# First tile of the first MLP by plain products over 384 tokens at once, and a new order of the filling steps

## What is computed

```python
def _attn_ref(q, k, v, tau):
    qn = q / (np.linalg.norm(q, axis=1, keepdims=True) + 1e-06)
    kn = k / (np.linalg.norm(k, axis=1, keepdims=True) + 1e-06)
    s = kn.transpose(0, 2, 1) @ qn / tau            # 256 x 256
    a = np.exp(s - s.max(-1, keepdims=True))
    a /= a.sum(-1, keepdims=True) + 1e-09
    return v @ a

x = _attn_ref(q, k, v, tau).reshape(6016, 256)
h = x @ moe_w_in                                    # 256 -> 2048
x = (h * np.cos(h)) @ moe_w_out                     # 2048 -> 256
h = x @ moe2_w_in
y = (h * (1.0 / (1.0 + np.exp(-h)))) @ moe2_w_out
```

## Time and profile before

| | |
|---|---|
| median of 3 executions | 1026.3 us (1025.75 to 1026.33) |
| the profiled execution | 1024.68 us |
| its span in the profile | 1022.9 us |
| PE busy, 8718 matmuls | 1017.5 us, 99% |
| DVE busy | 945.7 us, 92% |
| ACT busy | 801.4 us, 78% |
| POOL busy | 1.5 us |

### The profile page before, as it was taken

How to read it: one execution, slowest core, us unless ns; L and a number is a source line. 1 busy time by engine, 2 the same in 40 slices (tenths; PEclk the granted TensorE clock), 3 DMA queues, 4 the chain that set the end, 5 groups by cost and what they waited for, 6 DMA issues and landing times.

```text
span 1022.9 us, 21208 instructions
## 1 busy us (share of the span) xinstructions
PE 1017.5 (99%) x8718; PEld 1006.9 (98%) x8718; DVE 945.7 (92%) x1062; ACT 801.4 (78%) x873; POOL 1.5 (0%) x14
## 2 busy tenths in 40 slices
PE   9999999999999999999999999999999999999998
PEld 9969999999999999999999999999999999999998
DVE  7999899999999999998988689999999999999987
ACT  7778778788788787787777677877877877878785
POOL 0000000000000000000000000000000000000000
PEclk9999999999999999999999999999999999999999
DMA  8830011230331312304145401101101101101000
GB/s 274 289 121 22 2 57 38 98 135 21 114 115 41 114 52 85 135 22 165 37 165 237 169 18 37 31 12 42 40 5 43 41 2 42 42 1 42 22 22 21
DMA packets 18701, 76.03 MB, mean 74 GB/s; under 512 B 1840, under 2 KB 6448, under 8 KB 16560
## 3 DMA queue, kind: packets, MB, share of 16 engines
q1 hardware_dynamic: 18608, 74.72, 21.2%
HBM read 47.71 MB, written 27.00 MB: 73 GB/s over the span
## 4 chain that ended last, share of the span: by engine, by line
PE 92%; ACT 0%; issue 0%; DVE 0%; ACTq 0%
PE banks L1442 31%; PE banks L1446 31%; PE banks L1445 31%; PE banks L1499 0%; ACT g_hi L571 0%; ACT s_part L524 0%; DVE xo L1161 0%; ACTq L570 0%; ACT banks L516 0%; ACTq L523 0%
## 5 line engine op out<-in xcount | busy, mean ns | idle before, releaser
L1445 PE MATMUL banks<-g_lo,w1out 128*128 128x256 f32 (+1 forms) x768 | 212.5, 277 | 0.0
L1442 PE MATMUL banks<-g_hi,w1out 128*128 128x256 f32 (+1 forms) x768 | 212.4, 277 | 0.0
L1446 PE MATMUL banks<-g_hi,w1out 128*128 128x256 f32 (+1 forms) x768 | 212.3, 276 | 0.0
L1442 PE MATMUL banks<-xf_hi,h1w 128*128 128x256 f32 (+1 forms) x672 | 187.6, 279 | 1.1 <-ACT banks L516 0.6
L1446 PE MATMUL banks<-xf_hi,h1w 128*128 128x256 f32 (+1 forms) x672 | 185.9, 277 | 0.0
L1445 PE MATMUL banks<-xf_lo,h1w 128*128 128x256 f32 (+1 forms) x672 | 185.9, 277 | 0.0
L1445 PE MATMUL banks<-xf_lo,h2w 128*128 128x256 f32 (+1 forms) x672 | 185.9, 277 | 0.0
L1442 PE MATMUL banks<-xf_hi,h2w 128*128 128x256 f32 (+1 forms) x672 | 185.8, 277 | 0.0
L1446 PE MATMUL banks<-xf_hi,h2w 128*128 128x256 f32 (+1 forms) x672 | 185.8, 276 | 0.0
L1445 PE MATMUL banks<-g_lo,o2w 128*128 128x256 f32 (+1 forms) x670 | 185.2, 276 | 0.0
L1446 PE MATMUL banks<-g_hi,o2w 128*128 128x256 f32 (+1 forms) x670 | 185.2, 276 | 0.0
(11 more groups left out here) (149 smaller groups left out, 2305.9 us busy)
## 6 DMA issues: line engine op xcount, KB each, us to landing
w_scr<-w_split SPq DMA_DIRECT2D x8, 1792.0 KB, 7.5
qk_raw<-qk SPq DMA_DIRECT2D x23, 512.0 KB, 4.4
h2w<-w_scr SPq DMA_DIRECT2D x4, 1792.0 KB, 8.0
o2w<-w_scr SPq DMA_DIRECT2D x4, 1792.0 KB, 8.0
form<-v_tiles SPq DMA_DIRECT2D x11, 512.0 KB, 3.6
x_scr<-xo SPq DMA_DIRECT2D x11, 512.0 KB, 2.6
form<-x_scr SPq DMA_DIRECT2D x11, 512.0 KB, 4.2
y_tiles<-xo SPq DMA_DIRECT2D x10, 512.0 KB, 5.1
```

Of the source, the lines that this page charges most:

```text
L1442: nc.tensor.matmul(out, w_hi, m_hi, start=start, stop=False, skip_group_check=True)
L1445: nc.tensor.matmul(out, w_hi, m_lo, start=False, stop=False, skip_group_check=True)
L1446: return nc.tensor.matmul(out, w_lo, m_hi, start=False, stop=stop, skip_group_check=True)
```

## The change

**First tile on PE.** Steps 0 to 3 no longer use the scheme. A unit u (`first_hidden`) is one group e of one step: u = 2q + e. It computes the plain product over both blocks of channels (k) for all 384 tokens: each matmul takes both halves, as two runs of 192 columns, and its result has the same two runs in one bank. A unit is 2 (groups of 128 features) x 2 (k) x 3 passes = 12 matmuls and fills two banks, 2(u mod 3) and the next. It waits until the unit three before has been gated (`unit_gated`), or, for u < 3, until the fold has left the banks. `first_output` has four groups a step of 6 matmuls, also over 384 columns, in place of eight groups over 192. Units 6 and 7 end with one extra matmul of 128 columns into the part of a bank that the first tile leaves unwritten.

**First tile on ACT and DVE.** Each unit has turns, phase, sine and gate of its own over 768 elements, all against PSUM: `first_turns`, `first_phase`, `first_sine`, `first_gate`. s1, s2, s3, c22 and c12 do not exist in steps 0 to 3. `hi_of_g` and `lo_of_g` are as before. The form of the first tile has no sums: four blocks of it are split instead of seven.

**Weights.** Slot 0 of the weights is now needed in two parts too: a new tensor `w11`. ACT moves each half of a fold whole to `wr[f]` (`move_fold`), then takes high parts from there (`hi_11`, `hi_three`); DVE makes `lo_11`, `lo_three` and the four sums, all from SBUF. The sums of fold f, with `hi_sums` and `lo_sums`, are first read in tile 1, steps 4 to 7.

**The rest.** `wr0` and `wr1` move in SBUF, `FOLD_BANKS`, `X_BANKS` and `OUT_AT` get other bank numbers, semaphores that count steps of the scheme start at step 4, and SP's first `load_raw` waits for the first tile's outputs and splits too. The hand-written lists of the filling are new on all three engines. From step 8 on the order is as before.

The core of the diff (`...` marks what is left out):

```diff
-        X_BANKS = (5, 6, 7)
+        X_BANKS = (6, 7, 5)
...
+        def unit_banks(u):
+            return banks[:, 2 * (u % 3):2 * (u % 3) + 2, :, 0:N[0]]
...
-        FOLD_BANKS = [(0, 1), (2, 3), (6, 7), (5, 7)]
+        FOLD_BANKS = [(0, 1), (2, 3), (4, 5), (6, 7)]
...
+                        for m in range(PIECES):
+                            sp.wait_ge(w_lo_ready[m], 1)
+                        sp.wait_ge(out_done[0], STEPS)
+                        sp.wait_ge(out_done[1], STEPS)
+                        sp.wait_ge(w11_ready, STEPS)
+                        sp.wait_ge(wu_three_ready, STEPS)
                         sp.wait_ge(h1w_sums_ready[3], 1)
...
+                def move_fold(f, k):
+                    act.wait_ge(fold_ready[k], f + 1)
                     act.wait_ge(row_scale_ready, 1)
+                    nc.scalar.activation(fold_slots(wr[f], 2 * k, 2 * k + 2), bank(FOLD_BANKS[f][k]), ACT.Copy,
+                                         scale=row_scale[:, k:k + 1]).then_inc(fold_moved[k], 1)
...
+                def first_turns(u):
+                    act.wait_ge(unit_done, u + 1)
+                    if u >= 4:
+                        act.wait_ge(g_lo_ready, u // 2 - 1)
+                    nc.scalar.activation(work_int[:, unit_slots(u), :, 0:N[0]], unit_banks(u), ACT.Identity,
+                                         bias=0.25).then_inc(unit_turns, 1)
...
+                def lo_three(f):
+                    dve.wait_ge(wu_three_hi, f + 1)
+                    nc.vector.tensor_tensor(h1w[f][:, 1, 0:3, :, :], wr[f][:, 1:4, :, :], h1w[f][:, 0, 0:3, :, :],
+                                            ALU.subtract).then_inc(wu_three_ready, 1)
...
-                    if f == 3 and k == 1:
-                        pe.wait_ge(wu_slot7, 3)
-                        pe.wait_ge(h1w_raw_ready[2], 2)
...
+                def first_hidden(u):
+                    q, e = divmod(u, 2)
+                    pe.wait_ge(xf_ready, 1)
+                    if e == 0:
+                        pe.wait_ge(w11_ready, q + 1)
+                    pe.wait_ge(wu_three_ready, q + 1)
+                    if u < 3:
+                        pe.wait_ge(fold_moved[0], u + 1)
+                        pe.wait_ge(fold_moved[1], u + 1)
+                    else:
+                        pe.wait_ge(unit_gated, u - 2)
+                    for j in range(2):
+                        for k in range(KC):
+                            w_hi, w_lo = (h1w[q][:, part, 2 * k + e - 1, j, :] if k + e else w11[:, q, part, j, :]
+                                          for part in range(2))
+                            mm = three_passes(unit_banks(u)[:, j, :, :], w_hi, w_lo,
+                                              xf_hi[:, 0, 2 * k:2 * k + 2, 0:N[0]], xf_lo[:, 0, 2 * k:2 * k + 2, 0:N[0]],
+                                              k == 0, k == KC - 1)
...
                 fold(2, 0)
-                hidden(1, 0)
                 fold(2, 1)
-                hidden(6, 0)
...
+                first_hidden(0)
+                first_hidden(1)
+                first_hidden(2)
                 fold(3, 0)
...
                 fold(3, 1)
+                first_hidden(3)
+                first_hidden(4)
+                first_hidden(5)
+                first_output(0, (0, 1, 2))
+                first_hidden(6)
+                first_output(0, (3,))
+                first_output(1, (0, 1))
+                first_hidden(7)
                 hidden(1, 4)
```

More of the change, by code:

```diff
@@ L792, in _ @@
-                turns_ps(2)
-                hi_sums(3)
-                turns(2)
-                hi_of_form(1)
-                s1(3)
-                sine(2)
-                s2(3)
-                s3(3)
+                move_fold(0, 0)
+                move_fold(1, 0)
+                hi_11(0)
+                move_fold(0, 1)
+                hi_three(0)
+                move_fold(1, 1)
+                split_piece(2)
+                hi_three(1)
+                move_fold(2, 0)
+                hi_sums(0)
@@ L1367, in _ @@
-                phase(2)
-                lo_of_form(1)
-                gate_ps(2)
-                gate(1)
-                c22(3)
+                first_phase(2)
+                first_gate(1)
+                lo_sums(1)
+                first_gate(2)
+                lo_of_g(0)
+                first_phase(3)
+                lo_three(3)
+                first_phase(4)
+                first_gate(3)
+                lo_11(3)
+                first_phase(5)
+                first_gate(4)
+                lo_of_g(1)
@@ L1372, in _ @@
+                first_gate(5)
+                slot7(2)
+                first_phase(6)
+                lo_of_form(1)
+                first_gate(6)
+                lo_sums(2)
+                lo_of_g(2)
+                first_phase(7)
                 split_piece(2)
-                c12(3)
-                lo_of_g(1)
-                gate(2)
-                phase_ps(3)
+                first_gate(7)
                 c22(4)
                 two_of_form(2)
-                phase(3)
-                lo_of_g(2)
@@ new lines, in first_output @@
+                def first_output(q, groups):
+                    for g in groups:
+                        e, d = divmod(g, 2)
+                        if q == 0 and e == 0:
+                            pe.wait_ge(fold_moved[d], STEPS)
+                        if g == 0:
+                            pe.wait_ge(g_lo_ready, q + 1)
+                            pe.wait_ge(w_lo_ready[q], 1)
+                        for j in range(2):
+                            f, slot = 2 * j + e, 4 * (q % 2) + 2 * e + j
+                            cols = slice(d * P, (d + 1) * P)
+                            out = banks[:, x_bank(0, d), :, 0:N[0]]
+                            begin = q == 0 and e == 0 and j == 0
+                            end = q == STEPS - 1 and e == 1 and j == 1
+                            mm = three_passes(out, w1out[q][:, 0, f, cols], w1out[q][:, 1, f, cols],
+                                              g_hi[:, slot, :, 0:N[0]], g_lo[:, slot, :, 0:N[0]], begin, end)
+                        if e == 1:
+                            mm.then_inc(out_done[d], 1)
```

507 lines of the change are left out of this document (234 added, 273 removed).

## The result

The changed kernel takes 1014.98 us (median of four runs, 1014.92 to 1015.06), the kernel before 1026.03 beside it (1025.18 to 1026.33). The ratio is 0.9894, interval 0.9877 to 0.9911: faster by 1.1%, about 11 us. The forecast was 1018.5 with a range from 1016.3 to 1022.0, so the direction was right and the gain was larger than the range allowed. The two profiled executions are closer to the forecast: the span went from 1022.9 to 1013.1, which is 9.8 us, where the sum had 7.8. So there are two questions: where 2.0 us of the span came from, and where the medians have another 1.25.

A forecast was written before the change was run, and what follows sets the result against it. PE's matmul stream was taken as the bound, with DVE right behind; -6.4 us of work, -2.3 of old waits and +0.9 of new gave -7.8, so 1018.5 us from the 1026.3 median, range 1016.3 to 1022.0 (own range 1016.6 to 1020).

The forecast's parts named there:

- the sum: Whole kernel: -6.4 us of PE work, -2.3 of old waits, +0.9 of new waits, in all -7.8 us.
- The price of a 384: First tile on PE: each matmul of 384 columns takes 0.175 us from start to start, as in the attention stretch.
- rival 2: First tile on PE: the operand's gap makes two runs of each matmul, 0.223 us apiece; 1027.7 us, chance 4%.
- rival 3: First tile on PE: time goes by columns, so 4,608 more columns cost 2.1 us; 1027.1 us, chance 2%.
- The work and the waits that go: First tile on PE: fewer, wider matmuls gain 6.4 us with fillers counted; six waits for ACT's copies vanish, 2.3 us.
- Rival 4: Units 3 to 7: strict queues hold gates back, each unit waits for a bank; slower, 1028.8 us, chance 3%.
- rival 1: Filling stretch: DVE becomes the bound, keeps its 6.1 us idle, PE gains only 4.6 us; 1021.7 us, chance 23%.
- I allow 0.9 us of new waits: Filling stretch: PE waits in places for the nearly full DVE, 0.9 us, the term least known.
- The balance of idle time: DVE between 60 and 130 us: idle time falls from 6.1 to 2.9 us, so DVE is nearly the bound.
- Steps 4 to 7 keep their instructions: Steps 4 to 7: the same instructions in a new order, costed at 0 us.
- The folds keep their 16 matmuls: Folds on PE: the matmuls stay as they were, costed at 0 us.
- the median of before is 1026.3, so I predict 1018.5: Last step: the profiled 1024.7 us would come to 1016.9; the forecast starts from the median 1026.3, giving 1018.5.

The follow-up runs named there:

- e7: The changed kernel with four extra DVE operations of 512 elements between the first tile's gates, results unread: 1017.35 us, ratio 0.9922.
- e4: The changed kernel with eight extra DVE operations of 512 elements between the first tile's gates, results unread: 1021.11 us, ratio 0.9944.
- e1: The changed kernel with the first tile's output groups back at 192 columns, in twice as many matmuls: 1020.41 us, ratio 0.9939.
- e10: The changed kernel again, unedited, in a later session: 1016.57 us, ratio 0.9896.
- e2: The changed kernel with the hidden units' input products back at 192 columns, outputs still at 384: 1021.19 us, ratio 0.9942.
- e6: The changed kernel with both hidden units and output groups of the first tile back at 192 columns: 1024.98 us, ratio 0.9994.
- e5: The changed kernel again, unedited, in another session: 1015.79 us, ratio 0.9902.
- e3: The changed kernel with the first MLP's output groups of all later tiles also over both halves, 512 columns at once: 1029.72 us, ratio 1.0027.
- e9: The changed kernel with one more matmul of 64 columns behind the second MLP's last 192-column group: 1015.98 us, ratio 0.9896.
- e8: The changed kernel with first-tile outputs at 192 columns and a 64-column matmul behind the second MLP's last 192-column group: 1019.83 us, ratio 0.9941.
- e11b: The changed kernel with 64-column matmuls behind the second MLP's last 192-column group and the first MLP's last 384-column group: 1014.85 us, ratio 0.9891.

## Why the prediction was wrong

**What held.** The price of a 384 (0.1746 for 0.175), with the gap at no cost: rival 2 (0.223) and rival 3 (by columns) are refuted by the rows at 76 to 87 us. The work and the waits that go: the first tile's matmuls fell by 8.91 us where the terms said 6.6 + 2.3 = 8.9. Rival 4 did not come: no unit waited for its bank. DVE ends level with PE; e7 and e4 show that rival 1's mechanism stood right behind, since 0.4 us more of DVE's work would have begun it.

**The step that failed first: "I allow 0.9 us of new waits".** None came. The balance of idle time was right in direction (2.9 forecast, 1.7 found), and the step from there was wrong: I took an engine that is nearly full to mean an engine that is late in places. Three units' banks stand between PE and DVE's gates. That short delays of DVE therefore reach PE only when its total is larger than PE's is my reading, which no run tests by changing the banks. e4 and e7 show where the edge lies: about 0.4 us of added work is taken up, and what goes beyond costs its full length. I had given the lower end as zero, and the own range held it, so this is a term mis-sized by 0.9, within its bounds.

**The second: "Steps 4 to 7 keep their instructions" was costed at nothing.** They do keep them, but not their price: -0.58 us. The 256s between output groups of 192 columns go at 0.119 and between groups of 384 at 0.1145, and e1 brings 0.44 of the 0.58 back by widths alone. The rest of the line was luck in part: behind the last group the two profiles compared both had the short stretch, and an execution like e10's would have shown 26.40 us, only 0.15 less than before. "The folds keep their 16 matmuls" was costed at nothing too, and measured -0.46. By e2 and e6 the width of what follows is not the cause; it came with the new order, and the cause within the order is open. Together these are 1.0 us that no bound covered. They and the waits are the 2.0 us of the span.

**The third: "the median of before is 1026.3, so I predict 1018.5".** The step added 1.6 us to the sum because the profiled execution (1024.7) was faster than the median, as if that distance were a constant of the program. It is in large part a property of an execution: whether one or two stretches of 256s run at 0.1177. The profile that I summed from had the short stretch at 600 us; executions of the kernel before in all sessions lie between 1024.66 and 1028.31. These are 3.65 us, more than the three terms of the table for the changed kernel make (about 0.7 + 0.45 + 1.4), so something more varies in the kernel before. The changed kernel's first four all lie with the profiled quick one, so the medians are 11.05 apart and the spans 9.8. In the later sessions the medians were 10.2 (e5) and 10.65 (e10) apart. That the kernel before has part of its high times from the same stretches is likely by its likeness to e1 and e10, but no profile of one of its slower executions was taken, so for that kernel it is open.

With the three mended the sum is 1024.7 - 9.8 = 1014.9 for a quick execution and about 1016.7 for one with both long stretches, and all runs of the changed kernel lie between 1014.87 and 1016.77. It took both kinds of error to leave the range: the steps of the sum alone would have given 1026.3 - 9.8 = 1016.5, the base alone 1016.9, and both are inside.

One sum of a rival is off as well, without effect: for rival 4 the waits must come to 2.5 + 7.8 + 0.9 = 11.2 us, since the 0.9 of new waits is already in the 7.8; the prediction has 10.3.

## What to carry to other kernels

Price a matmul by the rows of its own size and its own neighbours. In this kernel 192 columns cost 0.1116 us where 128 x 128 weights are loaded for each, and 384 cost 0.1746, so pairs of narrow matmuls under one set of weights are where a wide operand pays; two of 256 (0.2268) against one of 512 (0.2328) have nothing left to win. An engine at 100% that feeds another through buffers need not cost anything, as here, where its total did not exceed the other's; weigh totals, and then test the edge with a known extra load, as the busy share cannot tell "level" from "late". An instruction that is taken away takes its margin with it: look at what waits behind it, as in e3. Count a stretch from its own start in the same execution; e1's 4.67 looked like the price to a hundredth and was two effects and an early start. And before adding a sum to a median, ask which kind of execution the profile was: one long stretch of equal matmuls, looked at in two profiles, tells it.

## What the runs showed of the hardware

- A stream of 256-column matmuls has two rhythms on the same data at full granted clock: 0.1133 and 0.1177 us (first profile and e10, 610 to 615 us). It goes in the slower one behind matmuls of 192 columns in every profile that has no small matmul there (598.6 to 602 us), and in some executions on to 642, or from 116 to 130 behind matmuls of 384 (e2, e9, e10). A single matmul of 64 columns ended it within four matmuls at 598.6 us in the three profiles that have it there (e8, e9, e11b); at 116 us one profile (e11b) cannot tell this from the short kind. Why it holds on, and what ends it by itself at 602 or at 642 us, is open.
- 256s between groups of 192 columns cost 0.1185 to 0.1196 us on average (before, e1, e6, e8), between groups of 384 0.1143 to 0.1147 (changed kernel, e2, e5, e9, e10, e11b).
- Prices from start to start at a granted clock of 1.00, each with its own weights: 64 columns 0.03 to 0.05 and 128 columns 0.05 to 0.06 when one stands alone (and a 256 behind it then takes 0.17 to 0.20), 192 in a row 0.1116 (before), 384 with a gap in the operand 0.1746 (changed kernel) and without one 0.175 (before), 512 0.2328 (e3). Groups of 192 among 256s go at 0.110 (e1).
- The first 55 us of this kernel differ by up to 0.4 us between three executions of one program (first fold at 55.44 to 55.87 us: changed kernel, e5, e10) and by 0.7 over all profiles (55.19 to 55.92), which moves everything behind them.
